# q and k loaded ahead of every weight, column norms placed among the last q-k products, softmax in two halves of its rows

## The reference

```python
qn = q / (norm(q, axis=1) + 1e-6)         # q, k, v: (1, 6016, 256); norms over the 6016 tokens
kn = k / (norm(k, axis=1) + 1e-6)
s = kn.T @ qn / tau                       # 256 x 256: attention over channels
a = exp(s - s.max(-1)); a /= a.sum(-1) + 1e-9
x = v @ a                                 # 6016 x 256
h = x @ w_in                              # 256 -> 2048
P = a0 + a1*h + a2*h**2 + a3*h**3
Q = 1 + |b0|*|h| + |b1|*h**2
x = (P / (Q + 1e-6)) @ w_out              # 2048 -> 256
h = x @ w_in2
out = (h * clip(h + 3, 0, 6) / 6) @ w_out2
```

## Time and profile before

| | |
|---|---|
| median of three runs | 1161.88 us |
| the profiled execution | 1161.6 us |
| its span, first to last instruction | 1159.6 us |
| PE busy | 1124.5 us, 97% of the span |
| DVE, ACT, POOL busy | 77%, 76%, 68% |
| the first slice product is in `H`, and ACT starts on it (L589) | 65.86 us from the span's start |
| PE busy from 300 to 1100 us | all of it but 0.4 us |

### The profile page before, as it was taken

One profiled execution on the slowest core, in us unless ns is written; L12 is line 12 of the kernel. 1 busy time (PEld: TensorE's weight loads), 2 busy tenths in 40 slices (PEclk: granted clock), 3 DMA queues, 4 the chain that ended last, 5 costly groups with the idle time before them and its releaser, 6 DMA issues.

```text
span 1159.6 us, 17859 instructions
## 1 busy us (share of the span) xinstructions
PE 1124.5 (97%) x5988; PEld 968.1 (83%) x5988; DVE 894.0 (77%) x1264; ACT 880.2 (76%) x1477; POOL 786.8 (68%) x628
## 2 busy tenths in 40 slices
PE   7888799999999999999999999999999999999998
PEld 6677588888888888888888888888888888888887
DVE  6779999887887887787787787787787787777621
ACT  6579888877877777787787787787787787787643
POOL 2248888776676676676676677677677677666643
PEclk9979899999999999999999999999999999999999
DMA  9851010010010010010010010000001000000000
GB/s 317 268 163 19 1 19 1 14 19 1 18 20 1 1 37 1 2 37 1 1 37 1 2 34 4 1 23 14 1 20 19 1 19 1 1 19 1 1 20 19
DMA packets 68377, 34.18 MB, mean 29 GB/s; under 512 B 51264, under 2 KB 61632, under 8 KB 68032
## 3 DMA queue, kind: packets, MB, share of 16 engines
q1 hardware_dynamic: 68288, 33.04, 10.1%
HBM read 26.87 MB, written 6.16 MB: 28 GB/s over the span
## 4 chain that ended last, share of the span: by engine, by line
PE 91%; DVE 5%; ACT 1%; issue 1%; POOL 0%; DMA 0%; SPq 0%; POOLq 0%; DVEq 0%; ACTq 0%
PE H L398 14%; PE H L399 14%; PE H L400 14%; PE OP L504 8%; PE OP L506 8%; PE OP L508 7%; PE YP L400 7%; PE YP L398 7%; PE YP L399 7%; PE OP L407 4%; DVE SQ L793 1%; DVE H L778 1%; DVE g_hi L786 1%; DVE T L771 1%; PE OP L444 1%
## 5 line engine op out<-in xcount | busy, mean ns | idle before, releaser
L356 POOL TENSOR_TENSOR SQ<-SQ,AB 128x512 f32<-128x512 f32 (+1 forms) x192 | 247.8, 1291 | 282.8 <-ACT SQ L591 282.3
L368 POOL TENSOR_TENSOR g_lo<-R,g_hi 128x512 fp32r<-128x512 f32 (+1 forms) x192 | 245.5, 1279 | 30.5 <-ACT g_hi L622 30.5
L362 POOL TENSOR_TENSOR g_lo<-SQ,Y 128x512 fp32r<-128x512 f32 (+1 forms) x192 | 245.4, 1278 | 5.0 <-DVE SQ L801 5.0
L589 ACT ACTIVATE AB<-H,absb 128x512 f32<-128x512 f32 (+1 forms) x192 | 130.2, 678 | 154.6 <-PE H L400 153.4
L504 PE MATMUL OP<-wd_hi,g_hi 128*128 128x256 f32 x752 | 211.7, 282 | 0.6 <-POOL g_lo L368 0.6
L506 PE MATMUL OP<-wd_lo,g_hi 128*128 128x256 f32 x752 | 211.9, 282 | 0.0
L771 DVE TENSOR_TENSOR T<-T,H 128x512 f32<-128x512 f32 (+1 forms) x192 | 129.4, 674 | 105.7 <-ACT T L597 105.5
L508 PE MATMUL OP<-wd_hi,g_lo 128*128 128x256 f32 x752 | 209.6, 279 | 0.0
L786 DVE SCALAR_TENSOR_TENSOR g_hi<-H,coef,Y 128x512 fp32r<-128x512 f32 (+1 forms) x192 | 141.6, 738 | 68.3 <-ACT Y L610 67.2
L398 PE MATMUL H<-vT_hi,wf_hi 128*128 128x512 f32 (+1 forms) x384 | 151.4, 394 | 13.9 <-DVE wf_lo L758 8.2
L793 DVE SCALAR_TENSOR_TENSOR SQ<-SQ,g_hi 128x512 f32<-128x512 f32 (+1 forms) x192 | 156.1, 813 | 6.6
(11 more groups left out here) (82 smaller groups left out, 2213.7 us busy)
## 6 DMA issues: line engine op xcount, KB each, us to landing
qk<-in_q SPq DMA_DIRECT2D x23, 256.0 KB, 7.8
qk<-in_k SPq DMA_DIRECT2D x23, 256.0 KB, 8.8
v_blocks<-in_v SPq DMA_DIRECT2D x88, 64.0 KB, 2.3
out<-o_tok SPq DMA_DIRECT2D x11, 512.0 KB, 3.0
wd_raw<-in_moe_w_out SPq DMA_DIRECT2D x8, 512.0 KB, 9.6
w_raw_a<-in_moe_w_in SPq DMA_DIRECT2D x1, 2048.0 KB, 14.5
wu_raw<-in_moe_w_in SPq DMA_DIRECT2D x4, 512.0 KB, 6.7
v_blocks<-in_v SPq DMA_DIRECT2D x8, 48.0 KB, 7.1
```

The costliest lines, as they stand in the source:

```text
L356: nc.gpsimd.tensor_tensor(SQ[:, j % 4, 0:w], SQ[:, j % 4, 0:w], AB[:, j % 2, 0:w], ALU.add)\
L362: nc.gpsimd.tensor_tensor(g1_lo[:, j % 4, 0:w], SQ[:, j % 4, 0:w], Y[:, j % 2, 0:w], ALU.mult)\
L368: nc.gpsimd.tensor_tensor(g2_lo[:, j % 4, 0:w], R[:, j % 2, 0:w], g2_hi[:, j % 4, 0:w].bitcast(fp32), ALU.subtract).then_inc(g2_lo_done, 1)
```

## The change

SP issues nothing but q's and k's loads, with block 0 of v behind load 12; all four parts of `wd1`, `w_raw_a`, block 1 of v and the later weights stand behind load 23. The first k load and the three small coefficient loads are issued by ACT. The absolute value and root of `b` move behind load 2, DVE's refinement of it behind load 3; v's block 0 is transposed by DVE behind load 14 and rounded by ACT behind load 16. ACT's four roundings of `wd1` stand around the root of the norms, POOL's four low halves wait until the squares are summed. DVE adds the two rows of `square_sum` itself, so PE needs four products for the norms, and these stand between loads 21 and 22, the spreading of the inverse between loads 22 and 23. Sums, roots and refined norms live in PSUM (`YP`). PE multiplies ones with ones nine times ahead of load 0 and six times behind load 23 (`keep_clock`). Each half of the softmax's rows is handed on alone: exponential, transposes, copy, fold.

```diff
-    W0_LOADS = 8, 12, 16, 20
+    V0_LOADED, V0_TRANSPOSED = 12, 14
+    NORMS_BEHIND, SPREAD_BEHIND = 21, 22
...
+        sums, roots = YP[:, 0, 0:4], YP[:, 0, 4:8]
+        inverse_q = small[:, 20:22]
... SP
-            sp.dma_start(coef[:, 0:4], a.partition_broadcast(P)).then_inc(consts_in, 16)
-            sp.dma_start(coef[:, 4:6], b.partition_broadcast(P)).then_inc(consts_in, 16)
-            sp.dma_start(coef[:, 6:7], tau.partition_broadcast(P)).then_inc(consts_in, 16)
                 sp.dma_start(qk[:, n % NQK, 0, 0:m, :], q_h[:, i:i + m, :]).then_inc(qk_in[n % NQK], 16)
-                sp.dma_start(qk[:, n % NQK, 1, 0:m, :], k_h[:, i:i + m, :]).then_inc(qk_in[n % NQK], 16)
-                if n in W0_LOADS:
-                    load_wd1(W0_LOADS.index(n))
+                if n >= 1:
+                    sp.dma_start(qk[:, n % NQK, 1, 0:m, :], k_h[:, i:i + m, :]).then_inc(qk_in[n % NQK], 16)
+                if n == V0_LOADED:
+                    load_v(0)
+            for part in range(4):
+                load_wd1(part)
             sp.dma_start(w_raw_a[:], w_up_h[0]).then_inc(w1_in, 16)
-            load_v(0)
             load_v(1)
... POOL
+            for c in range(CT):
+                vT_split(0, c, 0)
+            pool.wait_ge(square_rows_summed, 1)
             for part in range(4):
                 wd1_split(part)
-            for c in range(CT):
-                vT_split(0, c, 0)
... PE
+            def keep_clock(n):
+                for _ in range(n):
+                    nc.tensor.matmul(H[:, 3, 0:P], ones[:], ones[:], start=True, stop=True)
+            def norms():
+                pe.wait_ge(square_rows_summed, 1)
+                for x in range(2):
+                    for c in range(CT):
+                        done = nc.tensor.matmul(YP[:, 0, 2 * x + c:2 * x + c + 1],
+                                                square_sum[:, x, 0, c * P:(c + 1) * P], ones[:, 0:1],
+                                                start=True, stop=True)
+                done.then_inc(norms_summed, 1)
+            def spread_inverse():
+                pe.wait_ge(ident_ready, 1)
+                pe.wait_ge(inverse_ready, 1)
+                for c in range(CT):
+                    done = nc.tensor.matmul(YP[:, 1, c * P:(c + 1) * P], inverse_q[:, c:c + 1].to_broadcast([P, P]),
+                                            ident[:], start=True, stop=True)
+                done.then_inc(inverse_spread, 1)
+            pe.wait_ge(ones_ready, 1)
+            keep_clock(9)
...
                 done.then_inc(qk_multiplied, 1)
+                if n == NORMS_BEHIND:
+                    norms()
+                if n == SPREAD_BEHIND:
+                    spread_inverse()
+            keep_clock(6)
             for c in range(CT):
+                pe.wait_ge(exp_ready, c + 1)
                 for d in range(CT):
+                    done = nc.tensor.transpose(YP[:, c, d * P:(d + 1) * P], prob[:, c, d * P:(d + 1) * P], ident[:])
+                done.then_inc(probT_psum, 1)
             pe.wait_ge(w1_in, 16)
... PE, fold(0) and up1: a half of the fold waits for its half of probT, a half of up1 for its half of wf_lo
+                        pe.wait_ge(probT_ready, c + 1)
+                    if isinstance(t, int) and t == 0 and j in PIECE_AT:
+                        pe.wait_ge(fold_lo, CT * PIECE_AT.index(j) + c + 1)
... ACT, behind load 23
+            wd1_round(0)
+            wd1_round(1)
             act.wait_ge(norms_summed, 1)
+            nc.scalar.activation(roots, sums, ACT.Sqrt).then_inc(roots_taken, 1)
+            wd1_round(2)
+            wd1_round(3)
...
+            nc.scalar.activation(small[:, 34:36], small[:, 26:28], ACT.Identity, bias=EPS_SUM).then_inc(exp_summed, 1)
...
             fold_split(0)
+            nc.scalar.activation(small[:, 40:41], root_b1, ACT.Abs_reciprocal_sqrt)
... DVE
+            nc.vector.tensor_tensor(square_sum[:, :, 0, :], square_sum[:, :, 0, :], square_sum[:, :, 1, :], ALU.add)\
+              .then_inc(square_rows_summed, 1)
+            ratio, norm, norm_k = small[:, 12:16], YP[:, 0, 8:12], small[:, 16:18]
...
+                nc.vector.tensor_reduce(small[:, 24 + c:25 + c], prob[:, c, :], AX.X, ALU.max, negate=True)\
+            for c in range(CT):
+                dve.wait_ge(probT_psum, c + 1)
+                nc.vector.tensor_copy(probT[:, :, c * P:(c + 1) * P],
+                                      YP[:, c, 0:C].rearrange("p (d m) -> p d m", d=CT)).then_inc(probT_ready, 1)
                 if c == 0:
+                    dve.wait_ge(exp_summed, 1)
+                    nc.vector.reciprocal(inverse_sum, small[:, 34:36]).then_inc(sums_inverted, 1)
```

More of the change, by code:

```diff
@@ L542, in _ @@
                    .then_inc(qk_squared, 1)
-                if n in W0_LOADS:
-                    part = W0_LOADS.index(n)
-                    rows = slice(part * J // 4, (part + 1) * J // 4)
-                    act.wait_ge(wd1_in[part], 16)
-                    nc.scalar.activation(wd1_hi[:, rows, :], wd1_raw[:, rows, :], ACT.Copy).then_inc(wd1_hi_done, 1)
-            sums, roots = small[:, 0:4], small[:, 4:8]
+                if n == 2:
+                    act.wait_ge(consts_in, 48)
+                    nc.scalar.activation(absb[:], coef[:, 4:6], ACT.Abs).then_inc(absb_ready, 1)
+                    act.wait_ge(absb_ready, 1)
+                    nc.scalar.activation(root_b1, absb[:, 1:2], ACT.Sqrt).then_inc(absb_ready, 1)
+                if n == V0_TRANSPOSED + 2:
+                    for c in range(CT):
+                        vT_split(0, c, 0)
+            wd1_round(0)
+            wd1_round(1)
             act.wait_ge(norms_summed, 1)
-            nc.scalar.activation(roots, YP[:, 0, 0:4], ACT.Sqrt).then_inc(roots_taken, 1)
-            nc.scalar.activation(sums, YP[:, 0, 0:4], ACT.Copy).then_inc(roots_taken, 1)
+            nc.scalar.activation(roots, sums, ACT.Sqrt).then_inc(roots_taken, 1)
+            wd1_round(2)
+            wd1_round(3)
             for c in range(CT):
@@ L704, in _ @@
                                         squares[:, n % 2, :, 0:m, :], ALU.add).then_inc(qk_summed, 1)
-            sums, roots = small[:, 0:4], small[:, 4:8]
-            guard, ratio, norm, inverse = (small[:, 8 + 4 * i:12 + 4 * i] for i in range(4))
-            by_tau = small[:, 28:29]
-            by_k = small[:, 30:32]
-            dve.wait_ge(roots_taken, 2)
+                if n == 3:
+                    exact_root()
+                if n == V0_TRANSPOSED:
+                    for c in range(CT):
+                        v_transpose(0, c, 0)
+            dve.wait_ge(qk_summed, len(loads))
+            nc.vector.tensor_tensor(square_sum[:, :, 0, :], square_sum[:, :, 0, :], square_sum[:, :, 1, :], ALU.add)\
+              .then_inc(square_rows_summed, 1)
+            guard, by_k = small[:, 8:12], small[:, 30:32]
+            ratio, norm, norm_k = small[:, 12:16], YP[:, 0, 8:12], small[:, 16:18]
+            dve.wait_ge(consts_in, 48)
+            dve.wait_ge(roots_taken, 1)
             link(nc.vector.tensor_scalar(guard, roots, 1e-30, None, ALU.max))
@@ L716, in _ @@
             link(nc.vector.tensor_scalar(norm, norm, 0.5, EPS_NORM, ALU.mult, ALU.add))
-            link(nc.vector.reciprocal(inverse, norm))
-            dve.wait_ge(ident_ready, 1)
-            for c in range(CT):
-                done = nc.vector.tensor_scalar(diag[:, c, :], ident[:], inverse[:, c:c + 1], None, ALU.mult)
-            done.then_inc(diag_ready, 1)
-            dve.wait_ge(consts_in, 48)
-            link(nc.vector.reciprocal(by_tau, TAU))
-            link(nc.vector.tensor_scalar(by_k, inverse[:, 2:4], by_tau, None, ALU.mult))
+            nc.vector.reciprocal(inverse_q, norm[:, 0:2]).then_inc(inverse_ready, 1)
+            link(nc.vector.tensor_scalar(norm_k, norm[:, 2:4], TAU, None, ALU.mult))
+            link(nc.vector.reciprocal(by_k, norm_k))
             spread = probT[:, 0, :]
```

99 lines of the change are left out of this document (38 added, 61 removed).

## The result

The changed kernel took 1158.23 us (median of 20 runs, 1155.81 to 1161.9), the kernel before 1161.99 beside it (20 runs). The ratio is 0.9965, 95% interval 0.9957 to 0.9973: faster by 0.35%. 1151.2 was forecast, with a range that ended at 1155.0. The direction was right, and a gain of 10.4 us was about 3.8. The profiled execution took 1158.11 (span 1156.2).

A forecast was written before the change was run, and what follows sets the result against it. PE was taken as busy nearly throughout, so only the opening could move. Gains of 6.4, 3.5 and 0.45 us sum to 10.4, taking the profiled 1161.6 to 1151.2; own range 1150 to 1152.7, with rivals 1149.0 to 1155.0.

The forecast's parts named there:

- an earlier fold: Opening: the fold of the softmax's result would start at about 52.1 instead of 58.55, 6.4 us earlier.
- the fold to the first pass: From the fold's start to ACT's first pass over `H`: 3.8 us at full clock instead of 7.31, 3.5 earlier.
- When the sums are ready: q-k stage: all 24 loads of q and k squared and summed by 43.7 us.
- the price of the wait: At the norms: PE, with loads 22 and 23 queued behind, waits about 1.5 us for the sums, bounds 0 to 4.
- rival C: Between 50 and 58 us the clock falls anyway; fold and first slice lose about 3, total 1154.2; chance 0.10.
- q-k from 5.0: Start: PE's q-k products begin at about 5.0 us, 1.3 earlier than before and at full clock.
- the small passes to the inverse: Behind the norms' products: root and six small passes take 1.5 us, with the inverse ready at 46.3.
- no wait in piece 1: Behind the first pass: ACT's 0.45 us wait in piece 1 for a half-clock fold product goes away.
- Rival A: At the norms: the sums come in time, PE doesn't wait, `w_raw_a` holds the fold; gain 11.8, total 1149.8; chance 0.20.
- Rival B: Norms and softmax: two DVE reciprocals wait for POOL's passes, 1.2 us each on average; total 1153.6, to 1156; chance 0.14.
- Rival D: At the fold: `w_raw_a` is delayed by later DMAs sharing the engines, to 63.5; slower than before; chance 0.03.

The follow-up runs named there:

- e2: The changed kernel with the three coefficient loads issued behind the square of load 3 and the root of b behind load 8: 1157.82 us, ratio 0.9959.
- f1: The changed kernel with v's block 0 loaded behind `w_raw_a`, split behind the softmax, and the coefficient loads issued behind load 3's square: 1153.69 us, ratio 0.9931.
- f0: The changed kernel with v's block 0 loaded behind `w_raw_a` and transposed and split behind the softmax: 1156.70 us, ratio 0.9956.
- e5: The changed kernel with twelve more products of ones on PE ahead of the norms: 1155.66 us, ratio 0.9949.
- g1: The changed kernel with norms and spreading behind load 23, coefficient loads late and POOL's `vT_lo` behind the sums: 1156.24 us, ratio 0.9948.
- h2: f1 without the nine products of ones ahead of load 0: 1155.71 us, ratio 0.9942.
- e1: The changed kernel with v's block 0 issued piecewise behind loads 9 to 16 and transposed behind load 18: 1158.69 us, ratio 0.9963.

## Why the prediction was right in sign and wrong in size

The forecast was 6.4 from an earlier fold, 3.5 from the fold to the first pass and 0.45 behind it. Measured were -0.9, 3.4 and 1.0. So the sign was right by the second term, and in part by luck: the term that was to carry the gain came out as a small loss.

The failed step is "When the sums are ready": forecast 43.7, measured 48.29. The 4.6 us are three terms, read from the squares (forecast: load 8 at 16.0, so load 1 at 16.0 - 7 x 1.36 = 6.5 and load 12 at 21.4).

- *The first loads: 2.4.* Load 1 was squared at 8.87, not 6.5. I had counted the three coefficient loads as free once they were off SP. They weren't: e2.
- *Moved work in the squares' stream: 1.6, not priced at all.* From load 1 to load 8 it took 19.96 - 8.87 = 11.1, against 9.5 at my pace. Between the squares of loads 2 and 3 stand the absolute value, a table load and the root (10.48 to 13.05 instead of 1.33 apart), then DVE's refinement. From there DVE sets the stream's pace: nine adds in 11.86, which is 1.32 each, 1.23 of it busy, with ACT waiting 0.27 for it before each square. That is hardly faster than the 1.36 at which the loads came, so what DVE loses is hardly made good: the 1.33 in which it waited for ACT behind the table load (14.13), and its own refinement. In f1, where the same work stands behind load 8, it cost 1.5 there (23.84 - 17.02 = 6.8 for four loads, against 5.3). This I read from two traces; no run took it out.
- *v's block 0: 0.6.* From load 12 to 23 it took 19.7; my 11 x 1.36 + 2.5 + 0.6 + 1.0 is 19.1. The size was nearly right (f0, with v out of the stream, had its sums 4.1 earlier, 0.9 of it because load 1 came sooner; I had allowed 4.1 for v) and the picture wrong, so this was luck: I had 384 KB at the bandwidth of the earlier trace rows and a gap of about 1. In truth SP stood 8.57 us, the DMA ran dry, and POOL's `vT_lo` and DVE's adds got into each other's way (3.65 for the pair, against 1.95 when alone in f1), as the add of the earlier trace rows had warned for `wd1`.

The second failed term is the price of the wait, forecast as 1.5 with bounds 0 to 4. It was 2.68, within the bounds, but only because two errors offset each other: PE too was late. It got load 1 at 8.89 instead of about 5.9 and was ready for the norms at 45.67 instead of 42.2, so the count of its products back to back from 5.0 failed with the first loads. And I had let the clock stay up through the wait. The forecast was 8.4 from the sums to the fold; it took 11.2, and 8.0 when e5 kept PE busy. That is rival C's mechanism at another place: I looked for it ahead of the fold, where warm-up products stand, and not ahead of the norms, where they don't. 4.6 + 2.8 make the 7.4 by which the fold was late.

Right were: q-k from 5.0 (measured 5.00); the small passes to the inverse, 1.5 (50.25 to 51.70); the fold to the first pass, 3.8 (3.87), table load included; no wait in piece 1. The fold ran at full clock behind the six products of ones, but no run takes these away, so what they are worth is not shown. POOL's halves of `wd1` hid behind ACT (they ended at 57.65, POOL's first pass over `SQ` began at 64.47). Rival A did not come: load 23 was squared at 45.00. Rival B was wrong: a reciprocal took 0.18 with POOL busy, as with POOL idle. Rival D didn't happen, yet its margin was thinner than I said: `w_raw_a` was issued at 42.34 and landed 13.6 later, at 55.9 instead of 50.5, and in g1 and h2 it did hold the fold. That is a late issue, not D's mechanism: from issue to landing it took 13.4 to 15.0 in all kernels here, against 14.5 before. Behind the first pass the time fell by 1.0 instead of 0.45; over all kernels here this stretch was 1094.7 to 1096.4, so the difference is not to be read.

## What to carry to other kernels

Before a transfer is moved into a full DMA stream, price its issue as well as its bytes: here the engine that issued it stood still for 8.57 and 12.12 us, and all that it would have issued or computed next waited too. Before a wait is given to PE, price the low clock behind it (about 3 us here), and put queued products or idle ones into it. When a chain of small steps is moved off the start into a running stream, look for the engine that paces that stream. Here it was DVE, at 1.32 us a load against arrivals of 1.36, and little of its own extra passes, or of its wait for ACT, was made good.

## What the runs showed of the hardware

- Eight DMAs of 48 KB held their issuing queue 8.57 us on SP and 12.12 on ACT, most of it with the DMA engines full (shares of 1.02 to 1.13).
- Such DMAs amid q and k brought the full DMA engines from 387 to 404 GB/s down to 265 to 279 (e1).
- Three broadcasts of 3.5 KB in all, issued beside the first 512 KB loads, delayed load 1 by 0.6 to 3.1 us (7.33 to 8.87 with them, 5.82 to 6.72 without).
- After PE's 2.68 us of idling at the norms the granted clock was at 0.5, the level of 1.2 GHz, for some 6 us of busy work, and came back between 54 and 56. With products of ones in the wait (e5) it stayed at 1.00.
